# Loads of an expert's weights: one DMA of 2 MB, or four of 512 KB

## The chip, the cores and the metric

The kernel runs on one core of a Trainium2 chip. What is measured is device time in microseconds; several runs of a kernel are made, and their median is compared. The numbers of the profile come from one more execution, taken by the hardware profiler.

## The reference, cut to what matters

Three stages run one after the other on float32 data.

```python
# 1. two-sided attention: x (8, 8, 512, 64), state (8, 8, 32, 64) -> 4608 rows of 512
xread = softmax(scale * x @ state.T) @ state
sread = softmax(scale * state @ x.T) @ x
# 2. a dense layer with hard-swish
h = x @ w_in                                  # (4608, 512) @ (512, 2048)
x = (h * clip(h + 3, 0, 6) / 6) @ w_out       # (2048, 512)
# 3. a mixture of 8 experts, each row goes to one of them
e_idx = argmax(x @ w_gate)
for e in range(8):
    mask = e_idx == e
    h = maximum(x[mask] @ w1[e], 0)           # (512, 1024)
    out[mask] = gate_w * eom * (h @ w2[e])    # (1024, 512)
```

The change is in the third stage. The weights `w1[e]` and `w2[e]` of an expert are 2 MB each.

## The kernel before, in words

Attention and the dense layer are computed batch by batch, and their rows are scattered into buckets in DRAM, one bucket per expert. A table computed on the core then lists tiles of 128 rows: for each tile its expert, the place of its rows, and what is due with it. The expert stage walks over 38 tiles: four written out, then a loop whose turn has four tiles (`loops`, L446, its loop at L458), and a rest. Each engine runs its own copy of that walk with its own `body(t)`, and they meet in semaphores only.

Float32 products are made of three: every operand is split into a high part in fp32r and the remainder. For an expert's weights ScalarE copies the high part (`split_hi`, L1072, the copy is recorded at L1077) in four pieces of 128x1024 and VectorE subtracts (`split_lo`, L478, recorded at L483). Source of both are the buffers `raw1` (for `w1`) and `raw2` (for `w2`), target is one of two slots in `we`. There is one raw buffer for each, so the next load into it may be issued only when the last piece has been subtracted.

The way of one tile t, with its lines:
- SyncE gathers its rows into `xg` by four DMAs (`load_rows`, L574). VectorE transposes them (`turn_rows`, L1431), ScalarE makes the high part (`rows_hi`, L1102), VectorE the low one (`rows_lo`, L1421).
- TensorE multiplies with `w1` (`first`, L913; into `h_ps` for even tiles and `y_ps` for odd ones).
- ScalarE takes the ReLU into `expert_hid` (L1140), two halves. SyncE stores each half into `hidden` in DRAM (L601) and reads it back in another order into `hid_mv` (four DMAs, L609); VectorE transposes (`turn_hidden`, L1554), ScalarE and VectorE split it (`hidden_hi`, L1114; `hidden_lo`, L1561).
- TensorE multiplies with `w2` (`second`, L929), two tiles after `first`. VectorE scales (L1544), GpSimd scatters the rows to the output (L692).

The order on ScalarE's queue is written out in its `body(t)` (L1129): `rows_hi` of tile t+1, the ReLU of tile t, `hidden_hi` of tile t-1, then, if tile t-1 is an expert's second tile, the split of the next expert's `w2` and the load of `w2` of the one after it (`load_w2`, L1123, its DMA at L1126); then, if tile t is an expert's second, the same for `w1` (`load_w1`, L1117, its DMA at L1120). Whether and what is split and loaded is read from the table into registers (`entry`, L442, L444). Eleven loads are issued so by ScalarE. Three more are issued by SyncE: `w1` of the first expert (L546), `w2` of the first (L560), `w1` of the second (L591), behind which stand the gathers of tile 2.

The lines of the loads before, and the wait of the splits:

```python
wait(act, "w1_ready", n)
act.dma_start(raw1[:], w1[bass.ds(e, 1)].rearrange("o p k f -> p (o k f)")
              ).then_inc(sem("raw1_loaded"), 16)
...
wait(act, f"raw{w + 1}_loaded", 16 * (n + 1))
```

Of the kernel before, what the change touches and what calls it, by code (L numbers as in the profile page):

```python
# [39 lines left out]
def emit_kernel(nc, x_rows, x_t_dram, keys, w_in, w_out, gates, w1, w2, out):  # L40
# [36 lines left out]
    def at(name, offset, shape, dtype):  # L77
        return nc.alloc_sbuf_tensor_at(name, shape, dtype, offset=SBUF_BASE + offset)
# [4 lines left out]
    o = 131072  # L83
# [158 lines left out]
    raw2 = at("raw2", 131072, [P, KE * DM], F32)  # L242
# [12 lines left out]
    raw1 = at("raw1", raw1_at, [P, KD * F], F32)  # L255
# [20 lines left out]
    def sem(name):  # L276
        if name not in sems:
            sems[name] = nc.alloc_semaphore(name)
        return sems[name]
# [102 lines left out]
    def wait(eng, s, value):  # L382

        if isinstance(value, int) and value <= 0:
            return
        eng.wait_ge(sem(s), value)
# [82 lines left out]
    PIECES = 4  # L469
    PIECE = KD * F // PIECES  # L470

    def piece(n, i, part):
        return part * WPART + n * KD * F + i * PIECE
# [4 lines left out]
    def split_lo(eng, w, n, w_at, pieces=range(PIECES), signal=None):  # L478
# [7 lines left out]
        if signal is not None:  # L486
            ins.then_inc(sem(signal), 1)

    block = nc.Block()
    blk = block.__enter__()  # L490

# [2 lines left out]
    def _(sp):  # L494
# [48 lines left out]

        sp.wait_ge(sem("sr_ps"), B)
        sp.wait_ge(sem("lt_ps"), B - 1)
        sp.dma_start(raw1[:], w1[0].rearrange("p k f -> p (k f)")).then_inc(sem("raw1_loaded"), 16)  # L546


        sp.wait_ge(sem("pad_row_ready"), 2)
# [7 lines left out]
        sp.dma_start(buckets[E * CAP:E * CAP + P, :], pad_row[:]).then_inc(sem("pads_stored"), 16)  # L557

        sp.wait_ge(sem("h_ps"), KF * (B + 1))
        sp.dma_start(raw2[:], w2[0].rearrange("p j d -> p (j d)")).then_inc(sem("raw2_loaded"), 16)  # L560


        def tile_rows(t):
# [3 lines left out]
        def load_rows(t):  # L567
            place = t.slot % 2
            of_tile = tile_rows(t)

            if not (t.first or is_b(t.n, 1)):
                wait(sp, "xg_turned", t.n - 1)
            for j in range(STRIPS):
                sp.dma_start(xg[NS * j:NS * j + NS, place, :, :],  # L574
                             of_tile[:, P * j:P * j + P].rearrange("(s t) c -> t s c", t=NS)
                             ).then_inc(sem(f"xg_loaded{place}"), 16)
# [11 lines left out]
        sp.wait_ge(sem("second_ready"), 1)  # L588
        e = sp.value_load(table[0:1, T_NEXT, MT:MT + 1], min_val=0, max_val=E - 1)
        sp.wait_ge(sem("w1_ready"), 1)  # L590
        sp.dma_start(raw1[:], w1[bass.ds(e, 1)].rearrange("o p k f -> p (o k f)")).then_inc(sem("raw1_loaded"), 16)  # L591
        load_rows(Tile(0, 2))

        def body(t):
# [27 lines left out]

        loops(sp, body, all_loaded)

        sp.wait_ge(sem("raw1_loaded"), 16 * 2)
        sp.wait_ge(sem("raw2_loaded"), 16 * 2)


    @blk.gpsimd
# [321 lines left out]
    def _(act):  # L951
# [77 lines left out]
        def mlp_block(b, cols, tiles):  # L1029
            for j in range(KF + LAG):  # L1030
                if j < KF:
                    n = KF * b + j
                    wait(act, "h_ps", n + 1)

                    hid_free(act, b, j)
                    act.activation(hid[:, hid_at(b, j), 0:cols], h_ps[:, j % 2, 0:cols], ACT.Relu, bias=three  # L1036
                                   ).then_inc(sem("relu_ready"), 1)
                    side(b, 2 * j)
                    if is_b(b, B - 1) and j in SPLIT_IN:
                        split_in_hi(SPLIT_IN[j])  # L1040
                    if is_b(b, 0):
                        split_out(j)
                    wait(act, "swish_ready", n + 1)
                    act.activation(hid_hi[:, hid_at(b, j), 0:cols], hid[:, hid_at(b, j), 0:cols], ACT.Copy  # L1044
                                   ).then_inc(sem("hid_hi_ready"), 1)
                    if j >= LAG:
                        side(b, 2 * j + 1)
                else:
                    side(b, KF + j)
                    if is_b(b, B - 1):  # L1050
                        state_tokens(range(2 * (j - KF), 2 * (j - KF) + 2))
                    if is_b(b, B) and j == KF:

                        act.wait_ge(sem("h_ps"), KF * (B + 1))
                        split_hi(0, 0, 0, range(SPLIT_EARLY))
# [15 lines left out]

        def split_hi(w, n, w_at, pieces=range(PIECES)):  # L1072

            wait(act, f"raw{w + 1}_loaded", 16 * (n + 1))
            raw = (raw1, raw2)[w]
            for i in pieces:
                act.activation(we[:, bass.ds(w_at + piece(w, i, HI), PIECE)], raw[:, i * PIECE:(i + 1) * PIECE],  # L1077
                               ACT.Copy).then_inc(sem(f"w{w + 1}_hi"), 1)
# [12 lines left out]
        for half in range(HALF):  # L1091
            side(B + 1, half)
            if half in SPLIT_LATE:
                split_hi(0, 0, 0, (SPLIT_EARLY + SPLIT_LATE.index(half),))


        def rows_hi(t):
# [5 lines left out]
                           ).then_inc(sem("xg_t_hi"), 1)  # L1103

        split_hi(1, 0, 0)
        rows_hi(Tile(0, 0))

# [9 lines left out]
        def load_w1(e, n):  # L1117

            wait(act, "w1_ready", n)
            act.dma_start(raw1[:], w1[bass.ds(e, 1)].rearrange("o p k f -> p (o k f)")  # L1120
                          ).then_inc(sem("raw1_loaded"), 16)

        def load_w2(e, n):  # L1123

            wait(act, "w2_ready", n)
            act.dma_start(raw2[:], w2[bass.ds(e, 1)].rearrange("o p j d -> p (o j d)")  # L1126
                          ).then_inc(sem("raw2_loaded"), 16)

        def body(t):  # L1129

# [11 lines left out]
            if not t.first:  # L1142
                hidden_hi(t.plus(-1))
                if is_b(t.n, 1):
                    load_w2(entry(act, Tile(0, MT), T_NEXT, E - 1), 1)


                before_it = t.plus(-1)
                with act.If(split2 > 0):
                    n = entry(act, before_it, T_ORD, E - 1) + 1  # L1150
                    other = entry(act, before_it, T_OTHER, WSLOT)
                    first_tile = entry(act, before_it, T_FIRST, MT)
                    load = entry(act, before_it, T_LOAD)
                    e = entry(act, before_it, T_NEXT, E - 1)

                    if not is_b(t.n, 1):
                        wait(act, "y2_ps", first_tile)
                    split_hi(1, n, other)
                    with act.If(load > 0):
                        load_w2(e, n + 1)  # L1160
            with act.If(split1 > 0):
                n = entry(act, t, T_ORD, E - 1) + 1
                other = entry(act, t, T_OTHER, WSLOT)
                load = entry(act, t, T_LOAD)
                e = entry(act, t, T_NEXT, E - 1)
                wait(act, "hid2_ps", HALVES * t.n)
                split_hi(0, n, other)
                with act.If(load > 0):
                    load_w1(e, n + 1)
# [475 lines left out]
```

## Time and profile before

| | us |
|---|---|
| median of 3 runs | 1194.17 |
| lowest, highest | 1190.5, 1194.36 |
| the profiled execution, its own time | 1194.88 |
| its span, first to last instruction | 1193.1 |
| TensorE busy in the span | 1136.7 (95%) |
| VectorE, ScalarE, GpSimd busy | 642.7, 467.4, 76.8 |

The profiled execution's own time is 1.8 us longer than its span, for what lies around the first and the last instruction. Engines are PE (TensorE's matmuls), PEld (its weight loads), DVE (VectorE), ACT (ScalarE), POOL (GpSimd), SP (SyncE); a q behind the name stands for the engine's sequencer, which issues DMAs, reads registers and branches. DMA queue q1 is SyncE's, q10 is ScalarE's, q0 is GpSimd's, q8 and q14 fetch instructions. The attention and the dense layer take the span's first 700 us or so, the experts the rest.

### The profile page before, as it was taken

To read this page: it belongs to the slowest core of one execution; us is meant where nothing else is said; L and a number is where in the kernel's file an instruction comes from. 1 tells how busy PE (TensorE), PEld (TensorE's weight loads), DVE (VectorE), ACT (ScalarE), POOL (GpSimd) and SP (SyncE) were. 2 spreads that over 40 slices of the span, in tenths; PEclk is the share of its full clock that TensorE was granted. 3 is DMA by queue.
4 is the path that set the end of the run, shared out by engine and by line. 5 is a ranking of instruction groups with operands and counts; after the bars stand their busy time and mean duration, and the time that the engine had idled before them with its cause. 6 is when DMAs were issued, how large, how long until landed. Compare 5 with 4: busy or idle time off the path is not lost.

```text
span 1193.1 us, 20974 instructions
## 1 busy us (share of the span) xinstructions
PE 1136.7 (95%) x6358; PEld 892.0 (75%) x6359; DVE 642.7 (54%) x1247; ACT 467.4 (39%) x780; POOL 76.8 (6%) x96
## 2 busy tenths in 40 slices
PE   9999999999999999999999986989979999879996
PEld 7777777777777777777779875777858887757884
DVE  6675655646556556465554375555543444456532
ACT  4454444444344434443543333343432223345320
POOL 0000101001001010010010110001000000000100
PEclk9999999999999999999999988998989999989999
DMA  9200101102110111010100756766654445655542
GB/s 370 75 36 32 40 36 54 54 1 71 36 36 36 37 71 36 1 72 1 71 36 1 263 172 204 240 195 218 189 197 151 138 141 171 204 169 177 170 139 73
DMA packets 98819, 131.65 MB, mean 110 GB/s; under 512 B 13967, under 2 KB 75023, under 8 KB 94352
## 3 DMA queue, kind: packets, MB, share of 16 engines
q1 hardware_dynamic: 91360, 89.35, 23.3%
q10 hardware_dynamic: 1584, 23.07, 5.7%
q0 software_dynamic: 5760, 17.90, 3.9%
q8 instruction: 47, 0.77, 0.3%
q14 instruction: 68, 0.56, 0.1%
HBM read 85.86 MB, written 45.47 MB: 110 GB/s over the span
## 4 chain that ended last, share of the span: by engine, by line
PE 77%; issue 5%; DVE 5%; ACTq 4%; DMA 3%; ACT 3%; SPq 2%; DVEq 1%; POOL 0%; POOLq 0%
PE y_ps L856 32%; PE h_ps L838 15%; PE y_ps L929 10%; PE h_ps L913 6%; PE y_ps L913 5%; ACTq L444 3%; PE a_ps L813 2%; DVE we L483 2%; PE h_ps L828 2%; DMA hid_mv<-hidden 1%; ACT we L1077 1%; DMA hidden<-expert_hid 1%; PE a_ps L716 1%; SPq L609 1%; PE a_ps L797 1%
## 5 line engine op out<-in xcount | busy, mean ns | idle before, releaser
L856 PE MATMUL y_ps<-w_out_hi,hid_hi 128*128 128x512 f32 x544 | 218.6, 402 | 0.0
L856 PE MATMUL y_ps<-w_out_lo,hid_hi 128*128 128x512 f32 x544 | 213.0, 392 | 0.0
L856 PE MATMUL y_ps<-w_out_hi,hid_lo 128*128 128x512 f32 x544 | 212.6, 391 | 0.0
L929 PE MATMUL y_ps<-we,act_t_hi 128*128 (+1 forms) x608 | 187.7, 390 | 0.9 <-issue 0.9
L1367 DVE SCALAR_TENSOR_TENSOR hid<-hid,h_ps 128x512 f32<-128x512 f32 (+1 forms) x144 | 94.5, 656 | 168.2 <-ACT hid L1036 168.2
L838 PE MATMUL h_ps<-att_hi,mix 128*128 128x512 f32 x512 | 184.5, 403 | 0.1
L1036 ACT ACTIVATE hid<-h_ps,three 128x512 f32<-128x512 f32 (+1 forms) x144 | 95.4, 662 | 177.3 <-PE h_ps L838 153.9
L856 PEld LDWEIGHTS y_ps<-w_out_hi,hid_hi 128*128 128x128 f32 x544 | 102.1, 188 | 51.1 <-issue 30.4
L929 PEld LDWEIGHTS y_ps<-we,act_t_hi 128*128 128x128 f32 x608 | 114.1, 188 | 25.8 <-issue 1.3
L1376 DVE TENSOR_TENSOR hid_lo<-hid,hid_hi 128x512 fp32r<-128x512 f32 (+1 forms) x144 | 94.9, 659 | 70.5 <-ACT hid_hi L1044 70.1
L856 PEld LDWEIGHTS y_ps<-w_out_hi,hid_lo 128*128 128x128 f32 x544 | 102.2, 188 | 23.2
L913 PE MATMUL h_ps<-we,xg_t_hi 128*128 (+1 forms) x304 | 100.6, 413 | 18.9 <-DVE xg_t_lo L1421 10.8
L929 PE MATMUL y_ps<-we,act_t_lo 128*128 (+1 forms) x304 | 118.6, 390 | 0.0
L913 PE MATMUL y_ps<-we,xg_t_hi 128*128 x304 | 99.7, 410 | 19.7 <-DVE xg_t_lo L1421 13.4
L856 PEld LDWEIGHTS y_ps<-w_out_lo,hid_hi 128*128 128x128 f32 x544 | 102.3, 188 | 19.9
L838 PEld LDWEIGHTS h_ps<-att_hi,mix 128*128 128x128 f32 x512 | 96.1, 188 | 27.8 <-issue 7.0
L1044 ACT ACTIVATE hid_hi<-hid 128x512 fp32r<-128x512 f32 (+1 forms) x144 | 87.5, 608 | 66.8 <-DVE hid L1367 66.8
L838 PE MATMUL h_ps<-att_lo,mix 128*128 128x512 f32 x256 | 99.8, 390 | 0.0
L1554 DVE STREAM_TRANSPOSE act_raw<-hid_mv 128x512 f32<-128x512 f32 x76 | 49.6, 691 | 89.5 <-DMA hid_mv<-hidden 85.1
L483 DVE TENSOR_TENSOR we<-raw,we 128x1024 f32 (+1 forms) x55 | 63.8, 1220 | 43.4 <-ACT we L1077 43.4
L913 PEld LDWEIGHTS h_ps<-we,xg_t_hi 128*128 128x128 f32 x304 | 59.8, 199 | 35.0 <-issue 21.3
L913 PEld LDWEIGHTS y_ps<-we,xg_t_hi 128*128 128x128 f32 x304 | 59.2, 196 | 35.6 <-issue 22.0
(216 smaller groups left out, 1405.4 us busy)
## 6 DMA issues: line engine op xcount, KB each, us to landing
raw<-in_w ACTq DMA_DIRECT2D x11, 2048.0 KB, 8.5
hidden<-expert_hid SPq DMA_DIRECT2D x76, 256.0 KB, 2.2
hid_mv<-hidden SPq DMA_DIRECT2D x152, 128.0 KB, 2.9
xg<-buckets SPq DMA_DIRECT2D x164, 64.0 KB, 1.9
xb<-in_x_rows SPq DMA_DIRECT2D x8, 1024.0 KB, 4.9
x_t<-in_x_t SPq DMA_DIRECT2D x7, 1024.0 KB, 4.8
buckets<-pad_row SPq DMA_DIRECT2D x8, 774.0 KB, 7.9
raw<-in_w SPq DMA_DIRECT2D x3, 2048.0 KB, 7.7
```

The source lines that it names most:

```text
L444: return eng.value_load(table[0:1, column, bass.ds(t.n, 1)], min_val=0, max_val=max_val)
L483: ins = eng.tensor_tensor(we[:, bass.ds(w_at + piece(w, i, LO), PIECE)], raw[:, i * PIECE:(i + 1) * PIECE], we[:, bass.ds(w_at + piece(w, ...
L813: i = pe.matmul(mix_bank(a, n, g)[NS * q:NS * q + NS, :], keys_of(a)[D * g:D * g + D, q, :], w_in_raw[D * g:D * g + D, q, mix_columns(n)], ...
L838: i = pe.matmul(h_ps[:, j % 2, 0:cols], mix[:, m % SLOTS, g, n % GO, wp, :], (att1_hi, att1_lo)[tp][:, g, 0:cols], start=(g == 0 and k == ...
L856: i = pe.matmul(y_ps[:, t, :], (hid_hi, hid_lo)[hp][:, hid_at(b, j), t * P:(t + 1) * P], w_out_s[wp][:, j, :], start=(j == 0 and m == 0), ...
L913: i = pe.matmul(hid2_banks[slot % 2][:, h, :], xg_t[xp][:, slot % 2, k, :], we[:, bass.ds(w_at + (wp * WPART + k * F + h * BANK), BANK)], ...
L929: i = pe.matmul(y2_ps[:, slot % 2, :], act_t[hp][:, slot % 2, f, :], we[:, bass.ds(w_at + (wp * WPART + KD * F + f * DM), DM)], start=(f = ...
L1036: act.activation(hid[:, hid_at(b, j), 0:cols], h_ps[:, j % 2, 0:cols], ACT.Relu, bias=three).then_inc(sem("relu_ready"), 1)
L1044: act.activation(hid_hi[:, hid_at(b, j), 0:cols], hid[:, hid_at(b, j), 0:cols], ACT.Copy).then_inc(sem("hid_hi_ready"), 1)
L1367: dve.scalar_tensor_tensor(out=hid[:, hid_at(b, j), 0:cols], in0=hid[:, hid_at(b, j), 0:cols], scalar=6.0, in1=h_ps[:, j % 2, 0:cols], op0 ...
L1376: dve.tensor_tensor(hid_lo[:, hid_at(b, j), 0:cols], hid[:, hid_at(b, j), 0:cols], hid_hi[:, hid_at(b, j), 0:cols].bitcast(F32), ALU.subtr ...
L1554: dve.transpose(act_raw[:, slot % 2, h * 4:h * 4 + 4, :].rearrange("p f t -> p (f t)"), hid_mv[:, h, :, :].rearrange("p s (k f) -> p k s f ...
```

## The change

Each load becomes four DMAs over a quarter of the buffer's columns each: of every partition's 16 KB, 4 KB at a time. `PIECES` is 4, and `PIECE` is 1024 elements. Each piece increments the same semaphore by 16, and every wait on it asks for four times as much as before, so that a split still begins when the whole load is there. Order and places of all else stay.

```diff
+    def load_pieces(eng, w, raw, weights):
+
+        for i in range(PIECES):
+            eng.dma_start(raw[:, i * PIECE:(i + 1) * PIECE], weights[:, i * PIECE:(i + 1) * PIECE]
+                          ).then_inc(sem(f"raw{w + 1}_loaded"), 16)
+
...
-        sp.dma_start(raw1[:], w1[0].rearrange("p k f -> p (k f)")).then_inc(sem("raw1_loaded"), 16)
+        load_pieces(sp, 0, raw1, w1[0].rearrange("p k f -> p (k f)"))
...
-        sp.dma_start(raw2[:], w2[0].rearrange("p j d -> p (j d)")).then_inc(sem("raw2_loaded"), 16)
+        load_pieces(sp, 1, raw2, w2[0].rearrange("p j d -> p (j d)"))
...
-        sp.dma_start(raw1[:], w1[bass.ds(e, 1)].rearrange("o p k f -> p (o k f)")).then_inc(sem("raw1_loaded"), 16)
+        load_pieces(sp, 0, raw1, w1[bass.ds(e, 1)].rearrange("o p k f -> p (o k f)"))
...
-        sp.wait_ge(sem("raw1_loaded"), 16 * 2)
-        sp.wait_ge(sem("raw2_loaded"), 16 * 2)
+        sp.wait_ge(sem("raw1_loaded"), 16 * PIECES * 2)
+        sp.wait_ge(sem("raw2_loaded"), 16 * PIECES * 2)
...
-            wait(act, f"raw{w + 1}_loaded", 16 * (n + 1))
+            wait(act, f"raw{w + 1}_loaded", 16 * PIECES * (n + 1))
...
             wait(act, "w1_ready", n)
-            act.dma_start(raw1[:], w1[bass.ds(e, 1)].rearrange("o p k f -> p (o k f)")
-                          ).then_inc(sem("raw1_loaded"), 16)
+            load_pieces(act, 0, raw1, w1[bass.ds(e, 1)].rearrange("o p k f -> p (o k f)"))
...
             wait(act, "w2_ready", n)
-            act.dma_start(raw2[:], w2[bass.ds(e, 1)].rearrange("o p j d -> p (o j d)")
-                          ).then_inc(sem("raw2_loaded"), 16)
+            load_pieces(act, 1, raw2, w2[bass.ds(e, 1)].rearrange("o p j d -> p (o j d)"))
```

## Rows read from the trace of the kernel before

**Rows 1.** Windows view, expert stage: us, busy (x instructions) per engine, clock, DMA, GB/s

```profile
709.90:1182.00 472.10, 433.16 (x1823) 349.96 (x1824) 237.69 (x375) 157.22 (x238) 35.87 (x37) 0.96 0.57 179
```

**Rows 2.** Timeline of TensorE: start, us, operation [idle before it and what ended it]

```profile
743.57 1.22 PE L913 MATMUL y_ps<-we,xg_t_hi 128*128 x2 [6.30 <-issue]
...
757.64 0.72 PE L913 MATMUL h_ps<-we,xg_t_hi 128*128 x2 [1.11 <-DVE xg_t_lo L1421]
...
791.92 0.72 PE L913 MATMUL y_ps<-we,xg_t_hi 128*128 x2 [0.91 <-DVE xg_t_lo L1421]
...
808.08 1.21 PE L913 MATMUL h_ps<-we,xg_t_hi 128*128 x2 [4.83 <-DVE xg_t_lo L1421]
...
873.42 1.22 PE L913 MATMUL y_ps<-we,xg_t_hi 128*128 x2 [8.02 <-DVE xg_t_lo L1421]
...
1009.22 0.72 PE L913 MATMUL y_ps<-we,xg_t_hi 128*128 x2 [1.37 <-DVE xg_t_lo L1421]
...
1023.58 1.14 PE L913 MATMUL h_ps<-we,xg_t_hi 128*128 x2 [3.09 <-DVE xg_t_lo L1421]
...
1055.53 1.22 PE L913 MATMUL h_ps<-we,xg_t_hi 128*128 x2 [8.04 <-DVE we L483]
```

**Rows 3.** Timeline of ScalarE ahead of the stop that ends at 873.42

```profile
848.27 0.36 ACTq L1120 DMA_DIRECT2D raw<-in_w  x1
...
857.80 3.91 ACT L1077 ACTIVATE we<-raw 128x1024 f32 x4 [4.56 <-issue]
863.84 0.35 ACTq L1126 DMA_DIRECT2D raw<-in_w  x1
871.83 0.63 ACT L1102 ACTIVATE xg_t_hi<-xg_raw 128x512 fp32r<-128x512 f32 x1 [10.13 <-issue]
```

**Rows 4.** Line 444 on ScalarE, 852 to 857 us: ns min/median/max, first and last start

```profile
L444 ACTq TENSOR_LOAD <-table x4: 282/695/1322, 852.7 to 856.5; - x4
```

**Rows 5.** Line 458 on ScalarE, 864 to 872 and 903 to 907 us

```profile
L458 ACTq COMPARE_BRANCH x1: 50/50/50, 864.7 to 864.7; - x1
...
L458 ACTq COMPARE_BRANCH x1: 45/45/45, 903.7 to 903.7; - x1
L458 ACTq FUSED_REGOPS x1: 56/56/56, 906.7 to 906.7; - x1
```

**Rows 6.** Line 601, issue to landing: 1023 to 1026 us, then 820 to 822 us

```profile
DMA to landing us min/median/max: 6.4/6.4/6.5
...
DMA to landing us min/median/max: 2.1/2.1/2.2
```

**Rows 7.** Timeline of ScalarE ahead of the stop that ends at 1055.53

```profile
1042.08 0.60 ACT L1140 ACTIVATE expert_hid<-y_ps 128x512 f32<-128x512 f32 x1 [2.12 <-PE y_ps L913]
1045.57 1.23 ACT L1114 ACTIVATE act_t_hi<-act_raw 128x512 fp32r<-128x512 f32 x2 [2.90 <-DVE act_raw L1554]
```

**Rows 8.** Timeline of SyncE: its DMA issues, start and us

```profile
730.25 2.54 SPq L609 DMA_DIRECT2D hid_mv<-hidden  x4
...
875.91 1.88 SPq L574 DMA_DIRECT2D xg<-buckets  x4
```

**Rows 9.** Line 1126, the loads of w2 by ScalarE

```profile
L1126 ACTq DMA_DIRECT2D raw<-in_w x6: 343/352/2687, 730.2 to 1075.7; - x6
```

**Rows 10.** Timeline of VectorE: the rows of tile 2, no idle time before them

```profile
721.88 0.70 DVE L1431 STREAM_TRANSPOSE xg_raw<-xg 128x512 f32<-128x512 f32 x1
```

**Rows 11.** DMA queues (packets, MB, share), 864 to 868.8, then 868.8 to 870.5 us

```profile
q10 hardware_dynamic: 89, 1.46, 86.0%
...
q10 hardware_dynamic: 45, 0.62, 87.9%
q14 instruction: 2, 0.02, 2.3%
```

**Rows 12.** DMA queues, 738 to 740 us, while a load and the gate's DMA are in flight

```profile
q10 hardware_dynamic: 50, 0.77, 95.6%
q1 hardware_dynamic: 56, 0.01, 2.4%
```

## Prediction

> **What bounds the kernel now.** I read the windows view first, to see how much of the expert stage TensorE does not use: of 472.1 us it is busy 433.2 [rows 1], so about 39 us are there to be won, and nothing in the attention and MLP stage is touched by an edit that runs once or twice there. Then the timeline of TensorE, for where those 39 us lie: eight stops, from 0.9 to 8.0 us, hold 33.7 us of it [rows 2]; between them TensorE runs without a gap. Almost every stop ends with `xg_t_lo` of the next tile, and one with the last subtraction of the new weights (L483). Third, ScalarE's timeline around two such stops [rows 3]. There the reader is to see one queue in which everything stands in order: split the next expert's weights (L1077), wait until VectorE has subtracted the last piece, issue the load of the expert after it (L1120, L1126), and only then `rows_hi` of the next tile, without which TensorE cannot begin it. So whatever a load costs on ScalarE's queue stands ahead of the next tile. The load itself is early: its weights are split many tiles after it has landed. It matters by what it holds up.
>
> Four things stand behind a load in flight. ScalarE reads four or five entries of the table into registers ahead of a split; under a load the four shown take 0.28 to 1.32 us, where 0.28 is what one takes in calm [rows 4]. ScalarE's jump back at the end of a turn of four tiles needs two instruction fetches: from the branch to the next instruction it is 3.0 us in calm and 6.9 us (864.7 to 871.65, just ahead of the 871.83 of [rows 3]) when the load was issued 0.9 us before [rows 5]. The store of a tile's hidden rows lands after 6.4 us instead of 2.1 [rows 6]. And `hidden_hi`, behind that store and its way back, comes late: at 1045.57, though the last ReLU before it ended at 1042.68 [rows 7].
>
> **The change, part by part.** It does not start any split sooner: the split waits for all four pieces (64 instead of 16). What it adds is three DMA issues per load.
>
> Price of one more issue. The nearest row is four issues with a register in their address, 1.88 us in all [rows 8]; the single one takes 0.35 [rows 9], so the pitch is (1.88 - 0.35) / 3 = 0.51 and three more cost 1.5 us. Lower bound: the bare durations, 3 x 0.34 = 1.0. Upper bound: one issue was held 2.7 us [rows 9] while SyncE issued its four `hid_mv` beside it (2.54 us, [rows 8]); that is one load of eleven, and its hold is there before too. I take 1.5.
>
> SyncE's three loads (L546, L560, L591) are costed at nothing: the first two stand ahead of long waits for the rows' scatter, and behind the third the rows of tile 2 are turned without any idle time before them [rows 10]; without that cover it would be 1.5 us once. Longer landing of a load in pieces: nothing, by the same slack of many tiles.
>
> ScalarE's loop grows by some tens of instructions per turn. A further fetch in calm costs the 3.0 us of [rows 5] at most, and in stretches without a split ScalarE sits waiting for TensorE, so I take nothing, and at most 3 us once.
>
> Now the waits behind a load. In pieces the load's bytes are the same. What is at issue is how much of the load another queue has to let pass. The trace shows this: with the load's data beginning at 864.8, the fetch requested at about 865.2 got its first packet only after 868.8 and then two within 1.7 us, among 45 packets of the load [rows 11]; so the queues take turns packet by packet, but only behind a backlog already committed, four to five packets of 16 KB on that DMA engine. That they take turns is also seen where the gate's small packets and the load's stand 56 to 50 in one stretch of 2 us [rows 12]. Is the backlog bounded in bytes (some 80 KB) or in packets? In bytes, 4 KB packets change nothing, a late arrival still waits for nearly the rest. I take bytes, since other queues' packets of 0.5 and 2 KB run back to back, which a backlog of five packets would hardly carry. In that case a piece-wise load holds the others up exactly as before, only ScalarE reaches them 1.5 us later, so that each wait that lasts to the load's end swallows up to 1.5 us of the cost.
>
> The sum, stop by stop [rows 2]:
> - 743.6: two loads stand ahead of it, L1126 at 730.2 [rows 9] and the L1120 that follows in the same body: +3.0.
> - 757.6: +1.5 for L1126, -1.0 since one slow register load less falls into the flight: +0.5.
> - 791.9: the store behind the load ahead of the 757.6 stop lands as before, hence 1.5 earlier against TensorE; +1.5 -1.5 = 0.
> - 808.1: +1.5, less 1.1 for a register load: +0.4.
> - 873.4: ScalarE carries both loads (848.3 and 863.8) in one chain, +3.0; register load -1.1; the fetch, reached later, -0.3: +1.6.
> - 1009.2: +1.5 -0.3 = +1.2, of which I count +0.9, as this stop is short because TensorE had work left.
> - 1023.6: +1.5. 1055.5: the store behind the load ahead of the 1023.6 stop lands 1.5 earlier against TensorE: -1.5.
> - the last two loads are followed by no stop of [rows 2]: 0.
> Together +6.4, against the profiled execution's 1194.88 us (span 1193.1): 1201.3. That execution is 0.7 above the median of the three runs, 1194.17, so in their terms 1200.6. With 1.0 per load in place of 1.5 it is +3 or so; with the 3 us of one more fetch, +10.
>
> **Rivals.**
> A, the other sign. The backlog is bounded in packets, or ends with the transfer, so that with 4 KB packets what another queue waits for falls to about a quarter. For it: the turns of [rows 12], and that the fetch came into the middle of the load [rows 11]. Against it: the store of [rows 6] did wait to the load's end. Priced: a fetch's excess of 3.9 us falls to 1.0 (-2.9), the slow register loads' excess of an estimated 1.9 us per split (two near 1.3 and 1.1 for 0.28 each) to 0.5 (-1.4), and the late `hidden_hi` gives back all of its 2.9 us. By stop: 743.6 +3.0; 757.6 +1.5 -1.4 = +0.1; 791.9 is gone, -0.9; 808.1 +1.5 -1.4 and 2 us more for starting earlier, -1.9; 873.4 +3.0 -1.4 -2.9 = -1.3; 1009.2 gone, -1.4; 1023.6 +1.5; 1055.5 -2.9. Sum -3.8. After the stops of 3 us and more TensorE's first pair of matmuls takes 1.14 to 1.22 us, after the short ones 0.72 [rows 2]; an estimate of 1 us is given back by the stops that become short. 1194.2 - 5 = about 1189. It decides from where the saved wait per load exceeds the 1.5 us of issues. The Trainium skill speaks for this one: "DMA: Bandwidth & Descriptors", section "Queues, rings and completion order", says that a DMA engine takes the queues in turn and drains a whole packet of some 9 to 17 descriptors of one before it switches. By that rule a piece is its own turn and holds an engine for a quarter of the time, and the time would be rival A's. The trace agrees in part only: a fetch came in before the load's nine descriptors on an engine can have been through [rows 11].
>
> B, both by halves: the backlog shrinks to half, the waits give back about what the issues cost, and each stop moves by under 2 us in either sense. Halfway between +6.4 and -5 lies +0.7: 1194.9.
>
> That the change does not do what it says is hardly possible: the issues are written out, and their packets can be counted.
>
> **How the numbers follow.** My forecast case gets 0.42, A 0.33, B 0.25. A measurement of this kernel tells 0.3% (3.6 us) from no change. The forecast case ends slower by more than that nearly always (0.37) and else within it; A faster by more in 0.26, else within; B is within it in 0.14, and 0.05 and 0.06 outside. So faster 0.31, same 0.26, slower 0.43. The range takes A with 2 us more of matmuls at full pace, and the forecast with the 3 us of one more fetch: 1187 to 1204. The forecast case alone would be 1197 (1.0 per load) to 1204.
>
> **What would show it.** Right: ScalarE's queue shows four issues at L1126 and L1120 with 0.5 us between them and the stop at about 743 longer by 3 us; queue q10 has four times the packets, 4 KB each; the fetch of the turn under a load still takes 6 us or more from branch to next instruction; `hidden<-expert_hid` behind a load still lands after 6 us. Wrong: those two fall to 4 us or less, register loads under a load stay below 0.6 us, and the stops at 808, 873 and 1055 shrink by more than the first one grows. If the issues cost 0.35 us or less apart, or were held, the term of 1.5 is wrong.

## The result, and the profile after

The changed kernel took 1199.14 us in the median of its first nine runs (1195.35 to 1203.77), the kernel before 1193.85 beside it: ratio 1.0045, 95% interval 1.0028 to 1.0063. A second measurement of the same program (below, "again") gave 1197.76 and a ratio of 1.0034 (1.0021 to 1.0047). So the change costs some 4 to 5 us; I had forecast 6.4. The two profiles hold less than that: the first is of an execution of 1195.35 us, the fastest of the nine, the one of again of 1198.26 us, and the kernel before was profiled at 1194.88. Between the profiles there are thus 0.5 and 3.4 us to be explained.

The windows of the expert stage, from the first expert matmul to the end of the last; first the changed kernel's first profile, then "again":

```profile
707.60:1182.40 474.80, 434.07 (x1823) 350.67 (x1824) 237.89 (x375) 157.09 (x238) 36.01 (x37) 0.96 0.56 178
```

```profile
708.40:1185.30 476.90, 434.37 (x1823) 350.37 (x1824) 237.73 (x375) 157.12 (x238) 36.05 (x37) 0.96 0.56 178
```

Against [rows 1] the stage is longer by 2.7 and 4.8 us: TensorE is busy 0.9 and 1.2 us more at the same granted clock, 0.96, and idle 1.8 and 3.6 us more. The stage also began earlier than before, at 707.6 and 708.4 instead of 709.9. About 1 us of that is there in the kernel's first 300 us already, long before any edited line has run (the first is at 583 us), and comes and goes with the execution (-1.1 to +0.2 over all profiles of this study), so lengths of the stage say more here than ends of single profiles.

TensorE's stops in the changed kernel, timeline view, to be read against [rows 2]:

```profile
741.88 1.21 PE L919 MATMUL y_ps<-we,xg_t_hi 128*128 x2 [6.88 <-issue]
...
757.25 0.73 PE L919 MATMUL h_ps<-we,xg_t_hi 128*128 x2 [2.69 <-DVE xg_t_lo L1425]
...
806.92 1.21 PE L919 MATMUL h_ps<-we,xg_t_hi 128*128 x2 [3.69 <-DVE xg_t_lo L1425]
...
871.64 1.22 PE L919 MATMUL y_ps<-we,xg_t_hi 128*128 x2 [7.96 <-DVE xg_t_lo L1425]
...
1007.46 0.72 PE L919 MATMUL y_ps<-we,xg_t_hi 128*128 x2 [1.68 <-DVE xg_t_lo L1425]
...
1023.00 1.22 PE L919 MATMUL h_ps<-we,xg_t_hi 128*128 x2 [4.20 <-DVE xg_t_lo L1425]
...
1054.41 1.22 PE L919 MATMUL h_ps<-we,xg_t_hi 128*128 x2 [6.69 <-DVE we L483]
...
1091.85 0.72 PE L919 MATMUL y_ps<-we,xg_t_hi 128*128 x2 [1.49 <-DVE xg_t_lo L1425]
```

The reader is to see that seven of the eight stops are at the same places with the same releasers. The stop of 0.91 at 791.9 is gone and one of 1.49 at 1091.9 is new. ScalarE's queue ahead of the long stop, against [rows 3]:

```profile
855.49 3.91 ACT L1083 ACTIVATE we<-raw 128x1024 f32 x4 [3.63 <-issue]
861.53 1.84 ACTq L492 DMA_DIRECT2D raw<-in_w  x4
870.06 0.63 ACT L1108 ACTIVATE xg_t_hi<-xg_raw 128x512 fp32r<-128x512 f32 x1 [10.66 <-issue]
```

The four issues take 1.84 us where one took 0.35. Yet `rows_hi` follows 8.5 us after the first issue, and before it was 8.0: of 1.5 us added, 0.5 arrives. The rest is taken out of the jump back to the loop's start (line 458, against [rows 5]):

```profile
L458 ACTq COMPARE_BRANCH  x1: 50/50/50, 863.9 to 863.9; - x1
L458 ACTq FUSED_REGOPS  x1: 56/56/56, 869.9 to 869.9; - x1
```

6.0 us instead of 6.9. The other jumps made behind a load went from 7.0, 6.1 and 6.0 to 5.0, 5.2 and 5.5. The store of the hidden rows that waits behind the load of 1019 (against [rows 6]), the pair of stores at 807 behind another load, and the page's row of the loads' queue:

```profile
DMA to landing us min/median/max: 6.0/6.0/6.1
...
DMA to landing us min/median/max: 4.9/5.0/5.0
```

```profile
q10 hardware_dynamic: 6336, 23.07, 5.8%
```

6.0 instead of 6.4, and 4.9 to 5.0 where the kernel before has 6.5 to 6.9. Over the seven pairs of stores that stand behind a load it is 4.9 to 6.1 us instead of 6.0 to 7.6. The queue moves four times the 1,584 packets of before, for the same bytes. Of ScalarE's 141 register reads after 700 us, 7 took over 0.6 us where 13 had. So an issue cost what was forecast, and the waits behind a load were shorter. There are two readings of the second: the smaller packets let others pass (a weak form of rivals A and B), or ScalarE and the stores simply arrive 1.5 us later at a wait that ends with the load, as the forecast had it in part.

### The profile page after: what moved, and what is told of

It is laid out like the page before. It is cut to its first block, busy times and chain, and to the rows that moved or that the text cites. A ratio compares the mean times of both kernels' runs of the same rounds, so it can differ in the third digit from the quotient of the medians.

```text
span 1193.6 us, 21088 instructions
## 1 busy us (share of the span) xinstructions
PE 1135.6 (95%) x6358; PEld 890.8 (75%) x6359; DVE 642.6 (54%) x1247; ACT 467.0 (39%) x780; POOL 76.9 (6%) x96
## 4 chain that ended last, share of the span: by engine, by line
PE 76%; issue 6%; DVE 5%; ACTq 4%; DMA 3%; ACT 3%; SPq 2%; DVEq 1%; POOL 0%; POOLq 0%
PE y_ps L862 32%; PE h_ps L844 15%; PE y_ps L935 9%; PE h_ps L919 5%; PE y_ps L919 5%; ACTq L444 2%; PE a_ps L819 2%; DVE we L483 2%; PE h_ps L834 2%; ACTq L492 2%; DMA hidden<-expert_hid 1%; ACT we L1083 1%; DMA hid_mv<-hidden 1%; SPq L615 1%; PE a_ps L722 1%
## 5 line engine op out<-in xcount | busy, mean ns | idle before, releaser
L862 PEld LDWEIGHTS y_ps<-w_out_hi,hid_hi 128*128 128x128 f32 x544 | 102.1, 188 | 51.1 <-issue 30.4
```

The costliest lines, as they stand in the source:

```text
L862: i = pe.matmul(y_ps[:, t, :], (hid_hi, hid_lo)[hp][:, hid_at(b, j), t * P:(t + 1) * P], w_out_s[wp][:, j, :], start=(j == 0 and m == 0), ...
```

## The experiments

All ratios are against runs of the kernel before on the same chip, with 95% intervals. The expectations speak of theories. The first: the issues cost, and the waits behind a load are as before. The second: the issues cost, and smaller packets give a part back. The third and fourth are on w1_later, further down: its gain is the vanished instruction fetches, or it is the move of the load itself.

**again.** The changed kernel, unedited.

> The changed kernel once more, for a second profile of it and a closer time. Both theories: 1199 us, +5 over the kernel before. Theory 1 (issues cost, waits are as before): ScalarE's jump back behind a load takes 6 to 7 us and a hidden store behind a load lands after 6.4 us or more. Theory 2 (the issues cost 1.5 us per load, and the smaller packets give part of it back): the jump back 5 to 6 us, the store 5 to 5.8 us, as in the first profile.

Measured: 1197.76 us, ratio 1.0034 (1.0021 to 1.0047). Jumps behind a load 4.2, 5.8, 5.6 and 5.4 us. The second theory's 5 to 6 us held at three of the four jumps (the landing of the stores is not in this trace), but that doesn't yet tell the reason for the shorter waits.

**one_4k.** The packets of the change without its issues (from the kernel before; the weights are padded in DRAM so that no two 4 KB rows adjoin, and `raw` is seen as four quarters):

```
-            act.dma_start(raw2[:], w2[bass.ds(e, 1)].rearrange("o p j d -> p (o j d)")
+            act.dma_start(quarters(raw2), w2[bass.ds(e, 1), :, :, 0:PIECE].rearrange("o p k f -> p (o k) f")
```

> The kernel before with one DMA per load, whose rows are padded in DRAM so that its packets are 4 KB instead of 16 KB: the packet size of the change without its issues. Theory 1 (the cost is the issues, waits behind a load are bounded in bytes): as before, 1194 us, within 1. Theory 2 (small packets shorten what others wait for): 1189 to 1191 us, jump back behind a load 5 to 6 us where it was 6 to 7, hidden store 5 to 5.8 us. If the queue's commit is counted in packets outright: 1186 us or less, jump back 4 us.

Measured: 1196.20 us, ratio 1.0022 (1.0009 to 1.0034). Neither 1194 nor 1190: in this form small packets made it some 2.6 us slower. The source view of the w1 loads and the page's DMA row show two costs that come with them:

```profile
L1123 ACTq DMA_DIRECT2D raw<-in_w x5: 571/591/602, 741.7 to 1056.7; - x5
```

```profile
raw<-in_w ACTq DMA_DIRECT2D x11, 2048.0 KB, 10.2
```

One such issue takes 0.59 us instead of 0.36, and the load lands after 10.2 us where the page of before has 8.5. In return the jumps behind a load were 6.7, 5.6, 5.4 and 4.6 us instead of 7.0, 6.9, 6.1 and 6.0, and 7 register reads instead of 13 were over 0.6 us. So there is something in "small packets let others pass", but in this form it doesn't pay. TensorE's stop ahead of the new weights, 8.04 us at 1055.5 before, is 9.43 us here, the largest single growth. Whether the padding's odd row pitch shares in the slower load was not tried.

**four_16k.** The issues without the packets, first attempt (from the changed kernel, Q = 32):

```
-            eng.dma_start(raw[:, i * PIECE:(i + 1) * PIECE], weights[:, i * PIECE:(i + 1) * PIECE]
+            eng.dma_start(raw[Q * i:Q * i + Q, :], weights[Q * i:Q * i + Q, :]
```

> The changed kernel with four issues per load, each of 32 partitions instead of a quarter of every partition, so that packets stay 16 KB: the issues of the change without its packets. Theory 1: as the changed kernel, 1199 us. Theory 2: slower than the changed kernel by what small packets give back, 1202 to 1205 us, with the jump back behind a load at 6 to 7 us and the hidden store at 6.4 us or more.

Measured: 1231.12 us, ratio 1.0309 (1.0295 to 1.0323), far outside both. The page's DMA row:

```profile
raw<-in_w ACTq DMA_DIRECT2D x44, 512.0 KB, 8.8
```

A piece lands after 8.8 us where the change's pieces take 5.6, and queue q10's packets take 8.8% of the engines' time instead of 5.8%, for the same bytes. New stops of 8.74 and 6.13 us appear in front of the second layer, where TensorE had none. A piece of 32 partitions is slow, and so this is no control for the issues. The Trainium skill has a reason, "SBUF — State Buffer", section "Door 1: The DMA port swizzle": a transfer's rate depends on how many of 16 ports its partitions reach, and 32 adjoining ones reach eight. The trace agrees that such pieces are slow; which ports they used no view shows.

**eight_2k.** Eight pieces of 256 KB (`for i in range(2 * PIECES)`, waits doubled).

> Eight pieces per load of 256 KB in 2 KB packets: the issues of a load take about 3.8 us instead of 1.85. Theory 1: another 2.0 us at each of the six or seven places where a load stands ahead of a stop, 1209 to 1213 us. Theory 2: the same issues, but the waits of the others shrink once more, by a lesser step than from 16 to 4 KB: 1206 to 1209 us, jump back behind a load under 5 us.

Measured: 1215.71 us, ratio 1.0189 (1.0174 to 1.0205): 21.7 us over the kernel before, more than either theory. No register read of ScalarE was over 0.6 us any more, and the jumps behind a load took 4.3, 6.2, 4.6 and 4.7 us, in part less than in the changed kernel; none of it made up for the longer issues, 3.8 us per load. Why it is 2.7 us over the first theory's 1209 to 1213 stays open. The stop of [rows 2] at 743.6 is 11.8 us long here.

**issues_only.** Second attempt at the issues alone: 125 partitions and three times one.

```
+        cuts = (0, P - 3, P - 2, P - 1, P)
...
+            eng.dma_start(raw[cuts[i]:cuts[i + 1], :], weights[cuts[i]:cuts[i + 1], :]
```

> The four issues alone: per load one of 125 partitions and three of one partition each, so that packets stay 16 KB and nearly the whole load is one transfer as before. If the issues cost what I summed (1.5 us at each of the places where a load stands ahead of a stop) and the small packets give nothing back: as the changed kernel, 1198 to 1199 us. If the small packets of the change give back about half of it: 1201 to 1204 us, with the jump back behind a load at 6 to 7 us and the hidden store at 6.4 us or more. If the issues cost nothing and the change is slower for its longer transfers: 1194 us.

Measured: 1312.05 us, ratio 1.0976 (1.0945 to 1.1006). TensorE's timeline:

```profile
783.95 1.22 PE L936 MATMUL y_ps<-we,act_t_hi 128*128 x2 [22.19 <-DVE act_t_lo L1566]
```

A load's data now come in over some 20 us instead of 7, and everything that moves hidden rows waits beside it. It says nothing of the issues, and a great deal of partitions: cutting a transfer by partitions is not a neutral way to cut it. The trace shows what kind of slow this is. Queue q10 while one load's data come in, first here (1084.8 to 1104.5 us), then in the kernel before (1001.8 to 1008.3 us):

```profile
q10 hardware_dynamic: 135, 2.10, 27.1%
...
q10 hardware_dynamic: 144, 2.10, 87.7%
```

The same bytes keep the 16 DMA engines 27% busy instead of 88%: most of the engines have nothing of this load to do. The counts point the same way. Before, a load is 144 packets (1,584 / 11), its 128 rows and 16 more; here it is 136 (1,496 / 11), 128 rows and 8 more for four DMAs. If every engine that takes part adds one packet, the 125 rows went over five engines and each single row over one; that is an inference from the counts, as no view names the engines.

**two_8k.** Two pieces of 1 MB (`C = 2 * PIECE`, two issues).

> Two pieces per load, of 1 MB and 8 KB packets: one more issue (0.5 us) instead of three. Issues alone: a third of the change's cost, 1195.5 us. With half of it given back by smaller packets: 1194 to 1197 us, not below the kernel before. From four_16k's surprise (pieces of few partitions are slow) nothing is expected here, as each piece has all 128 partitions.

Measured: 1195.95 us, ratio 1.0017 (0.9999 to 1.0035), inside the expected 1194 to 1197, where the issues alone (1195.5) lie too, so it doesn't tell the theories apart. With 1, 2, 4 and 8 pieces the cost is 0, about 2 (the interval just includes 0), 4 to 5, and 22 us: slow at first, then steep.

**one_large_piece.** Four issues whose packets stay large, with all 128 partitions in each piece:

```
+        cuts = (0, 3712, 3840, 3968, 4096)
...
+            eng.dma_start(raw[:, cuts[i]:cuts[i + 1]], weights[:, cuts[i]:cuts[i + 1]]
```

> The control that four_16k and issues_only did not give, as their pieces were narrow: four issues per load, each over all 128 partitions, of 3712, 128, 128 and 128 of the 4096 columns. So ScalarE's queue carries the change's issues and its code, while nine tenths of the load still go in packets of 14.8 KB. If the change's cost is its issues and smaller packets give nothing back: as the changed kernel, 1197 to 1199 us. If 4 KB packets give back about half of what the issues cost: 1201 to 1204 us, register reads under a load at 0.6 us and more as often as in the kernel before (13 on ScalarE), the jump back behind a load at 6 to 7 us. Under 1196 us would say that the issues themselves cost next to nothing and the change's cost lies in its packets.

Measured: 1198.50 us, ratio 1.0038 (1.0024 to 1.0051), the changed kernel's time. Its ScalarE timeline and its line 458 around the jump of [rows 5]:

```profile
863.41 1.93 ACTq L493 DMA_DIRECT2D raw<-in_w  x4
872.16 0.63 ACT L1109 ACTIVATE xg_t_hi<-xg_raw 128x512 fp32r<-128x512 f32 x1 [10.90 <-issue]
```

```profile
L458 ACTq COMPARE_BRANCH  x1: 50/50/50, 865.9 to 865.9; - x1
L458 ACTq FUSED_REGOPS  x1: 56/56/56, 872.0 to 872.0; - x1
```

With nine tenths of the load in packets of 14.8 KB, the jump is 6.1 us (changed kernel 6.0), the others 5.2, 5.3 and 5.4 (5.0, 5.2, 5.5), and 6 register reads are over 0.6 us (7). The pair of stores that before took 6.4 us [rows 6] lands here after

```profile
DMA to landing us min/median/max: 4.7/4.7/4.8
```

and the seven pairs after 4.4 to 6.5 us (4.9 to 6.1). So in the change the shorter waits don't need the small packets: they are there with large ones. ScalarE comes 1.5 us later to a wait that ends about when the load does: counted from the load's first issue, the first instruction behind the jump of [rows 5] came after 7.8 us before, 8.4 in the changed kernel and 8.6 here. Only one_4k departs from this, with 6.7. The cost of the change is the issues and their code, and its packets neither add to it nor give anything back that this can tell; by the intervals of the three ratios, 1 or 2 us either way would not show.

**w1_later.** Does it matter where on ScalarE's queue a load is issued? From the kernel before, one DMA per load:

```
                     e = entry(act, before_it, T_NEXT, E - 1)
+                    with act.If(load > 0):
+                        load_w1(e, n + 1)
...
-                load = entry(act, t, T_LOAD)
-                e = entry(act, t, T_NEXT, E - 1)
                 wait(act, "hid2_ps", HALVES * t.n)
                 split_hi(0, n, other)
-                with act.If(load > 0):
-                    load_w1(e, n + 1)
```

> The kernel before with the load of w1 moved by one body: from behind split_hi(0), where it waits for VectorE's last subtraction and stands ahead of rows_hi, to the next body's block ahead of split_hi(1), where that wait is long over. If what delays TensorE is what stands ahead of rows_hi on ScalarE's queue: the stops at 808, 1009 and 1104 shrink or go and those at 743 and 873 lose little, 1188 to 1192 us. If the traffic of the load decides (fetches, stores), it is only moved: 1193 to 1195, or slower where it now falls on the split of w2 and the jump back.

Measured: 1165.39 us, ratio 0.9753 (0.9724 to 0.9782). That is 28 us, where I had hoped for 2 to 6 (the profile is of the fastest of six runs, 1161.63). TensorE's windows row of the stage, ScalarE's timeline at the place of [rows 3], and the page's row of the instruction queue:

```profile
707.70:1148.30 440.60, 425.09 (x1821) 345.49 (x1822) 237.30 (x375) 156.35 (x238) 35.95 (x37) 0.98 0.60 192
```

```profile
843.00 3.91 ACT L1077 ACTIVATE we<-raw 128x1024 f32 x4 [3.82 <-PE y_ps L929]
849.04 0.34 ACTq L1126 DMA_DIRECT2D raw<-in_w  x1
850.08 0.63 ACT L1102 ACTIVATE xg_t_hi<-xg_raw 128x512 fp32r<-128x512 f32 x1 [3.18 <-issue]
```

```profile
q14 instruction: 32, 0.26, 0.1%
```

From the load's issue to `rows_hi` it is 1.0 us instead of 8.0: the jump back fetches nothing any more. Six jumps of line 458, at 801 to 1019 us, each take 0.3 us, and queue q14 moves 32 packets in the whole kernel, not the 68 of before, with none between 801 and 1121 us. Moving the load had removed two register reads per tile from ScalarE's code, and so the turn of four tiles had become one that is held without fetching. TensorE's idle time in the stage fell from 38.9 to 15.5 us, its busy time by 8.1, at a granted clock of 0.98 instead of 0.96.

**w1_later_pieces.** The same move in the changed kernel.

> The same move in the changed kernel, with four pieces per load. If an issue costs only where it stands ahead of rows_hi: w1's issues still stand ahead of split_hi(1) and its rows_hi, so +4 to +6 us over w1_later, as the change cost before. If the wait for w1_ready hid a part of the issues' cost before, more: +6 to +9 us over w1_later.

Measured: 1184.36 us, ratio 0.9909 (0.9881 to 0.9937), 19 us over w1_later, not 4 to 9. The page's row of the instruction queue:

```profile
q14 instruction: 69, 0.57, 0.2%
```

In this kernel the pieces cost some four times what they cost in the other, and the fetches are back: the jumps behind a load take 4.5 and 5.1 us.

**w1_later_dead.** Is it the code? To w1_later is added, per tile, code that never runs (and the bound given for one register read is raised, so that the condition isn't known to be false):

```
+                    with act.If(load > 1):
+                        for _ in range(18):
+                            act.activation(spare, three, ACT.Copy)
```

> w1_later with code that is never executed: behind the load of w2, under a condition that is never true, 18 ScalarE instructions per tile. In w1_later queue q14 carries 32 packets of instructions instead of 68, and ScalarE's jump back takes no time. Theory 3 (w1_later wins because its turn of four tiles is short enough to need no fetches, and the move of the load is the lesser part): the fetches are back, q14 at 65 to 70 packets, the jump back 3 us in calm and 4 to 6 us behind a load, and the time 1180 to 1190 us. Theory 4 (the move itself wins): 1165 to 1168 us.

Measured: 1170.05 us, ratio 0.9790 (0.9759 to 0.9821). The page's row of the instruction queue:

```profile
q14 instruction: 69, 0.57, 0.2%
```

The fetches are back as expected, the first two jumps take 6.4 and 5.8 us, and a stop of 3.67 us stands at 859.2 where w1_later has none:

```profile
859.20 0.73 PE L913 MATMUL y_ps<-we,xg_t_hi 128*128 x2 [3.67 <-DVE xg_t_lo L1422]
```

But the time lies between the theories' numbers: instructions that are never executed cost some 4.7 us here, not 15 to 20. The two kernels ran on different chips and the intervals of their ratios overlap (0.9724 to 0.9782, 0.9759 to 0.9821), so the size of this is uncertain, but not that it is far from 15. The move of the load, with the two register reads per tile that it saves, is then worth some 22 us even with the fetches in place; the move and the reads were not tried apart. My third theory had the fetches right and the price wrong.

This also splits the 19 us of w1_later_pieces. Against w1_later_dead, where one DMA per load runs beside the same 69 packets of fetches, it is some 14 us slower: TensorE is idle 30.4 us of the stage instead of 18.9, and busy 433.0 instead of 429.2. So most of the 19 is the pieces themselves, and some 5 the fetches.

**before_hoist.** The other way round: the load stays, the code shrinks.

```
+            if PEEL <= t.c < PEEL + RING - 1:
+                kept[t.c] = of_split(t)
...
-                    n = entry(act, before_it, T_ORD, E - 1) + 1
-                    other = entry(act, before_it, T_OTHER, WSLOT)
+                    n, other, load, e = kept.pop(before_it.c, None) or of_split(before_it)
```

> The kernel before, the load in its place, but with fewer ScalarE instructions in a turn: in three of the four tiles the four entries of the table are read once, ahead of the ReLUs, and not in each of the two split blocks. Theory 3: it needs no fetches either, q14 at about 32 packets, 1160 to 1172 us. Theory 4: as before but for some us of register reads taken from the path ahead of a split, 1185 to 1192 us, with the jump back still at 6 us behind a load.

Measured: 1170.92 us, ratio 0.9811 (0.9774 to 0.9847), in the third theory's range. TensorE's timeline where [rows 2] has five stops of 1.4 to 8.0 us:

```profile
802.64 0.72 PE L913 MATMUL h_ps<-we,xg_t_hi 128*128 x2 [1.26 <-DVE xg_t_lo L1423]
...
1032.41 1.21 PE L913 MATMUL h_ps<-we,xg_t_hi 128*128 x2 [8.60 <-DVE we L483]
```

q14 carries 32 packets again, the jumps from 805 to 1033 us take 0.3 us. The stops of 8.0 us at 873.4, of 1.4 at 1009 and of 3.1 at 1024 are gone. ScalarE's timeline at the place of [rows 3] shows two savings side by side:

```profile
847.16 3.90 ACT L1077 ACTIVATE we<-raw 128x1024 f32 x4 [0.64 <-PE y_ps L929]
854.25 0.35 ACTq L1126 DMA_DIRECT2D raw<-in_w  x1
855.30 0.63 ACT L1102 ACTIVATE xg_t_hi<-xg_raw 128x512 fp32r<-128x512 f32 x1 [4.24 <-issue]
```

Without the fetches `rows_hi` follows the load's issue after 1.0 us instead of 8.0. And the register reads, which in three of four tiles now stand ahead of the ReLUs instead of ahead of the split of w2, no longer hold that split: its idle time is 0.64 us instead of 4.56. How the 22 us divide between the two was not separated.

**w1_later_hoist.** Both edits.

> Both: the load of w1 moved and the entries read once. Theory 3: no fetches are left to save, only the register reads and the wait on w1_ready: 1158 to 1166 us, no more than 5 us under the better of w1_later and before_hoist. Theory 4: 1155 to 1162 us.

Measured: 1163.16 us, ratio 0.9738 (0.9709 to 0.9768), with w1_later the fastest version of this study. Alone, w1_later saves 28 us (22 with the fetches in place) and before_hoist 22, together 29. The savings don't add up, as both edits shorten the same chain on ScalarE's queue ahead of the same stops; of the stops of [rows 2] the one at 1055.5 is left nearly whole, as 7.98 us at 1025.7.

## Why the prediction came out as it did

The direction was right, and so was the mechanism: the issues cost time on ScalarE's queue, and the size of the packets matters little. The size, 6.4 for 4 to 5, is nearly right, but in good part by luck: the eight stops that were to bring all of it brought +0.1 and +1.4 us in the two profiles. By its steps:

- **The price of an issue.** Forecast (1.88 - 0.35) / 3 = 0.51 per further issue; measured four in 1.83 to 1.85 us. Right.
- **The stop at 743.6, +3.0.** Wrong in size: +0.6 and +1.3 in the two profiles. I counted L1126's hold of 2.7 us [rows 9] as staying and put 1.5 on top. In its place four issues took 2.35 and 2.37 us altogether, less than the one held issue had:

```profile
727.41 2.35 ACTq L492 DMA_DIRECT2D raw<-in_w  x4
732.34 3.90 ACT L1083 ACTIVATE we<-raw 128x1024 f32 x4 [5.00 <-issue]
738.38 1.84 ACTq L492 DMA_DIRECT2D raw<-in_w  x4
740.32 0.63 ACT L1108 ACTIVATE xg_t_hi<-xg_raw 128x512 fp32r<-128x512 f32 x1 [4.08 <-issue]
```

- **The waits behind a load last as long as the load, in bytes.** Right for the change, by one_large_piece: with packets of 14.8 KB or 4 KB the jumps, the stores and the register reads come out alike. Not right for every form of load, by one_4k: counted from the load's issue, the instruction behind the jump came 0.1 to 1.1 us sooner than before, though the load lands after 10.2 us instead of 8.5. What I undersized is how much of the 1.5 us such a wait swallows. I took 0.3 us for a jump reached 1.5 us later; the four jumps behind a load were shorter by 2.1, 0.9, 0.9 and 0.4. So 873.4 moved by -0.1 and +0.2 instead of +1.6, and 1009.2 by +0.3 and +0.7 instead of +0.9.
- **The other stops.** Forecast, then the two profiles: 757.6 +0.5, +1.6, +1.2; 791.9 0, and it is gone (-0.9) in both; 808.1 +0.4, -1.1, +0.1; 1023.6 +1.5, +1.1, -0.4; 1055.5 -1.5, -1.4, -0.7. All eight: +6.4 forecast, +0.1 and +1.4 measured.
- **"The last two loads are followed by no stop: 0".** Wrong: a stop of 1.49 (1.46) us at 1091.9 is new. And I had read [rows 2] as if TensorE ran without a gap between its eight stops. The kernel before has three more: 3.13 us at 718.8, 0.93 at 1176.7, and one behind the last two loads,

```profile
1103.78 0.73 PE L913 MATMUL h_ps<-we,xg_t_hi 128*128 x2 [1.20 <-DVE xg_t_lo L1421]
```

which became 0.5 shorter. The new stop and this one make +0.9 together. The remainder of the stage's +2.7 and +4.8 is 0.9 and 1.2 us of busy time and changes of under 0.6 us each in the other two stops and in small gaps. So the total came near the forecast with smaller terms in more places; 6.4 was not confirmed term by term.
- **SyncE's three loads, taken as nothing.** Nothing is seen of them: the stop at 718.8, the first behind the third of them, is 3.13 and 3.28 us.
- **The signs I named.** Four issues with 0.5 us between them and four times the packets came as said. "The stop at about 743 longer by 3 us" did not, "6 us or more" from branch to next instruction held at one of the four jumps, and "after 6 us" at one of the seven pairs of stores.
- **Rival A** (waits fall to a quarter, 1189) is out: the time went the other way, and no jump under a load (4.2 us and more) and no store behind one (4.9 and more in the first profile) fell to 4 us. Its page, "DMA: Bandwidth & Descriptors" of the Trainium skill, "Queues, rings and completion order", has an engine drain a whole packet of 9 to 17 descriptors before it takes another queue. One_large_piece against the changed kernel shows no gain from smaller turns. One_4k shows a smaller one than the rival's, and eight_2k no register read over 0.6 us; none of it paid for its issues. **Rival B** (half, 1194.9) had the waits shorter, as seen, but by half, and by the size of the packets: over the 3.0 us in calm [rows 5] the four jumps had 3.5 us in the mean before and 2.4 after, and one_large_piece has the same with large packets.
- **A further fetch: 0 to 3 us, taken as nothing.** Right here, q14 has 70 packets after 68. (Nor does every jump need the two fetches of [rows 11]: at 1001.3 and 1055.8 the trace of before has one packet each.) But I had priced the instruction fetches as a given of the kernel. They can be removed, and [rows 5] showed where they stand: 6 to 7 us at each jump under a load, in front of long stops. What they are worth is known in w1_later only, some 4.7 us; in the kernel before it was not measured apart from the register reads.

Open: how much of the change's 4 to 5 us is the time of the issues and how much their code. One_large_piece carries both. Against it being the code alone speaks that the fetches are hardly more (70 to 68).

## What to carry to other kernels

Cutting a load into pieces is not free when the queue that issues it also feeds the bottleneck engine: count the issues ahead of the next tile's work, not the bytes, and let what waits to the load's end anyway absorb a part. Before tuning what stands around a loop's jump, look whether the jump fetches instructions at all, by the packets of the instruction queue and by the time from branch to next instruction: here three register reads fewer per tile in ScalarE's code (before_hoist), or one load issued a block later with two reads fewer (w1_later_dead), were each worth some five times what the whole change cost. And when an experiment cuts a transfer, cut it along the columns and leave all 128 partitions in each piece; cut by partitions it becomes another transfer.

## What the runs showed that I had not expected

- **Fetches come or go with a small change of the code.** 32 packets on q14 in w1_later, before_hoist and w1_later_hoist, 68 to 80 in all others that were profiled; the jump back takes 0.3 us in the first and 3 us in calm, 4 to 9 us under a load, in the others. 18 never-executed instructions per tile bring the fetches back. The Trainium skill speaks of this in "Runtime: NRT & Kernel Launch", section "Instruction fetch mechanics": a taken branch whose target is outside the window of two pages that an engine holds has to fetch it by DMA first. The trace agrees that such a jump fetches or doesn't as the code grows; whether the loop's length decides or where it lies against the pages, no run here separates.
- **The same three issues cost 4 to 5 us in one kernel and 19 in another** that was 28 us faster. Some 5 us of the 19 are the fetches that came back, by w1_later_dead; the other 14 are the pieces. That the faster version has less slack, so that more of each issue reaches TensorE, is a reading that no run here tests.
- **Narrow pieces are slow:** 32 partitions +37 us, 125 + 1 + 1 + 1 partitions +119 us, with the same bytes and the same four issues as one_large_piece's +5.
- **A DMA of 512 rows of 4 KB** takes ScalarE 0.57 to 0.60 us to issue, one of 128 rows of 16 KB 0.34 to 0.36.
